# The second layer of a fused attention and two-layer MLP: runs of 512, 512, 512, 384, 384 tokens per half, with moving rows 512 words apart

## The reference

```python
p_packed = sm_attn(p, k, v)            # 8 x 8 heads, 32 packed rows, 576 keys, 64 wide
out = sm_attn(q, p_packed, p_packed)   # back to 576 rows
x = out as [4608 tokens, 512]
h = x @ w_in                           # 512 -> 2048
y = (max(h, 0) + alpha * min(h, 0)) @ w_out        # 2048 -> 512
g = y @ w_gate; val = y @ w_val                    # 512 -> 1536 each
result = (g / (1 + exp(-g)) * val) @ w_down        # 1536 -> 512, moe2_w_out
```

## Time and profile before

| | us |
|---|---|
| median of 3 runs | 1641.13 (1640.57 to 1642.71) |
| profiled execution, its own time | 1641.77 |
| its span, first to last instruction | 1640.0 |
| TensorE busy | 1610.9 (98%) |
| VectorE busy | 1016.4 (62%) |
| ScalarE busy | 694.3 (42%) |

### The profile page before, as it was taken

How to read it: one execution, slowest core, us unless ns; L and a number is a source line. 1 busy time by engine, 2 the same in 40 slices (tenths; PEclk the granted TensorE clock), 3 DMA queues, 4 the chain that set the end, 5 groups by cost and what they waited for, 6 DMA issues and landing times.

```text
span 1640.0 us, 24546 instructions
## 1 busy us (share of the span) xinstructions
PE 1610.9 (98%) x9510; PEld 1492.1 (91%) x9510; DVE 1016.4 (62%) x1888; ACT 694.3 (42%) x1481; POOL 47.4 (3%) x81
## 2 busy tenths in 40 slices
PE   8999999999999999999999999999999999999999
PEld 5999988999999999999988888888999999999998
DVE  5776679867798768877544464445444644464443
ACT  4565568455675557645412141213212422242122
POOL 0000001100000000010000000000000000000000
PEclk9999999999999999999999999999999999999999
DMA  7343225432333324344364525443545354434541
GB/s 261 118 124 112 68 84 166 157 113 87 125 102 123 132 72 143 112 156 149 113 226 135 178 93 182 155 160 114 174 165 180 113 200 158 160 113 156 180 135 45
DMA packets 99731, 227.05 MB, mean 138 GB/s; under 512 B 9744, under 2 KB 41504, under 8 KB 99616
## 3 DMA queue, kind: packets, MB, share of 16 engines
q1 hardware_dynamic: 91136, 194.02, 36.4%
q0 software_dynamic: 8480, 31.47, 5.0%
HBM read 184.56 MB, written 40.89 MB: 137 GB/s over the span
## 4 chain that ended last, share of the span: by engine, by line
PE 81%; DVE 13%; ACT 3%; issue 2%; DMA 0%; SPq 0%; ACTq 0%; DVEq 0%
PE acc L874 9%; PE acc L666 8%; PE acc L668 8%; PE acc L667 8%; PE h L666 7%; PE side L666 7%; PE h L668 7%; PE h L667 7%; PE side L668 7%; PE side L667 7%; PE acc L878 5%; DVE piece L1294 3%; DVE mixed L1294 2%; DVE floats L1479 2%; DVE g L1294 1%
## 5 line engine op out<-in xcount | busy, mean ns | idle before, releaser
L874 PE MATMUL acc<-g,w 128*128 128x288 f32 x1792 | 272.4, 294 | 0.0
L874 PEld LDWEIGHTS acc<-g,w 128*128 128x128 f32 x1792 | 248.9, 188 | 0.0
L989 ACT ACTIVATE g<-floats 128x288 fp32r<-128x288 f32 x256 | 113.8, 445 | 224.5 <-DVE floats L1479 136.7
L1294 DVE TENSOR_TENSOR g<-floats,g 128x288 fp32r<-128x288 f32 x256 | 115.2, 450 | 76.5 <-ACT g L989 75.2
L666 PE MATMUL h<-attn,mixed 128*128 128x288 f32 x512 | 157.9, 308 | 3.5 <-DVE floats L1479 2.2
L1479 DVE SCALAR_TENSOR_TENSOR floats<-floats,h 128x288 f32<-128x288 f32 x256 | 130.5, 510 | 46.0 <-ACT floats L1148 44.3
L878 PE MATMUL acc<-g,w 128*128 128x288 f32 x896 | 156.0, 296 | 0.2 <-DVE g L1294 0.2
L667 PE MATMUL h<-attn,mixed 128*128 128x288 f32 x512 | 151.2, 295 | 0.0
L668 PE MATMUL h<-attn,mixed 128*128 128x288 f32 x512 | 151.2, 295 | 0.0
L1294 DVE TENSOR_TENSOR piece<-floats,piece 128x512 fp32r<-128x512 f32 (+3 forms) x203 | 135.8, 689 | 23.1 <-ACT piece L989 20.7
L1294 DVE TENSOR_TENSOR u<-sums,u 128x448 fp32r<-128x448 f32 (+1 forms) x120 | 76.7, 639 | 92.5 <-ACT u L989 92.5
(11 more groups left out here) (257 smaller groups left out, 3686.0 us busy)
## 6 DMA issues: line engine op xcount, KB each, us to landing
ring<-w_scratch SPq DMA_DIRECT2D x90, 512.0 KB, 5.5
ring_c<-w_scratch SPq DMA_DIRECT2D x60, 512.0 KB, 5.0
w_scratch<-piece POOLq DMA_DIRECT2D x36, 512.0 KB, 4.0
floats<-w_in SPq DMA_DIRECT2D x64, 256.0 KB, 3.2
ring_b<-w_scratch SPq DMA_DIRECT2D x30, 512.0 KB, 6.7
y_scratch<-floats POOLq DMA_DIRECT2D x16, 576.0 KB, 3.5
floats<-kT SPq DMA_DIRECT2D x28, 288.0 KB, 2.9
floats<-qT SPq DMA_DIRECT2D x28, 288.0 KB, 2.9
```

What stands on the lines that cost most here:

```text
L874: pe.matmul(acc[:, m, 0:CH], w2[:, j, x, m * P:(m + 1) * P], g[:, s % 2, 0, :], start=False, stop=False)
L989: return nc.scalar.activation(dst, src, ACT.Copy, **kw)
L1294: return nc.vector.tensor_tensor(dst, x, high.bitcast(F32), ALU.subtract)
```

## The change

1. `HALF` becomes 512, 512, 512, 384, 384 (before: 480, 480, 448, 448, 448). `HW` becomes 512, so every row of the moving operands of the second layer starts at a multiple of 512 words from the first tensor.
2. To make room, the order of the tensors is changed, the last down tile (`down_last`) and one scratch row (`value2`) move to the place of the raw buffers in `floats`, `ostage` and `yraw` begin 256 and 128 words earlier, and the fourth part of the ring's even set (`ring0_b`) takes the place of the twelfth down tile.
3. The waits follow the places. The fourth part of the weights of set 0 is loaded from slot 254 on, behind the last load of down weights, and waits for the output tile of slot 251. The split of the last down tile waits until all splits before it are done, in place of the output tile of slot 251. The first `out_copy` also waits for all splits.

```diff
-HALF = [480, 480, 448, 448, 448]
+HALF = [512, 512, 512, 384, 384]
...
-MID[LAST + 1] += [("yload",), ("wload",)]
+MID[LAST + 1] += [("yload",), ("wload", range(3))]
+MID[SLOTS - 2].append(("wload", range(3, 4)))
...
-            down_ = later("down", NT2 * 1024)
+            down_ = later("down", (NT2 - 1) * 1024)
+            ring0_b = later("ring0_b", 1024)
             ring1_ = later("ring1", 4096)
             blocks_a = later("blocks_a", 4 * 4 * HW)
+            sums_ = later("sums", (NT2 + 4) * HW, F32)
+            blocks_b = later("blocks_b", 3 * 4 * HW)
             ring0_a = later("ring0_a", 512)
-            sums_ = later("sums", 8192, F32)
-            blocks_b = later("blocks_b", 3 * 4 * HW)
-            ring0_b = later("ring0_b", 1024)
             u_ = later("u", 4 * HW)
             later("pad", 256)
             silus_ = later("silus", 1152, F32)
             ring0_c = later("ring0_c", 2048)
+            down_last = later("down_last", 1024)
+            value2_ = later("value2", HW, F32)
...
-        yraw = f(4224, 2 * KD * HW).rearrange("p (k c n) -> p k c n", k=KD, c=2)
-        ostage = f(2304, KD * HW).rearrange("p (m n) -> p m n", m=KD)
+        yraw = f(4096, 2 * KD * HW).rearrange("p (k c n) -> p k c n", k=KD, c=2)
+        ostage = f(2048, KD * HW).rearrange("p (m n) -> p m n", m=KD)
...
-            def load_weights(n):
+            def load_weights(n, parts=range(4)):
...
-                for i in range(4):
+                for i in parts:
                     if n == 1:
                         once.wait_ge(y_done, SLOTS - 3 + i)
                     elif n == 0 and i == 3:
-
-                        once.wait_ge(h_done, SLOTS - NT1)
+                        once.wait_ge(y_done, SLOTS - 4)
...
+                elif p == ("d", NT2 - 1):
+
+                    once.wait_ge(piece_split, n)
                 elif p[0] == "d":
                     once.wait_ge(y_done, SLOTS - NT1 + p[1] + 1)
...
                     if o == 0:
                         once.wait_ge(y_stored, 16 * NCH)
+                        once.wait_ge(piece_split, len(PIECES))
```

More of the change, by code:

```diff
@@ L249 @@
 RINGED = [p for p in PIECES if p[0] in "kvqwgs"]
+assert RAW_NO["d", NT2 - 1] % RING in (2, 3)
 LEAVE_NO = {p: n for n, p in enumerate(p for e in PLAN for p in pieces_of(e))}
@@ L371, in down @@
         def down(j):
-            return down_[:, 1024 * j:1024 * j + 1024].rearrange("p (x n) -> p x n", x=2)
+            t, a = (down_, 1024 * j) if j < NT2 - 1 else (down_last, 0)
+            return t[:, a:a + 1024].rearrange("p (x n) -> p x n", x=2)
         def block_of(name):
@@ L377, in block_of @@
             return t[:, 4 * HW * a:4 * HW * (a + 1)].rearrange("p (x k n) -> p x k n", x=2, k=2)
-        yraw = f(4224, 2 * KD * HW).rearrange("p (k c n) -> p k c n", k=KD, c=2)
-        ostage = f(2304, KD * HW).rearrange("p (m n) -> p m n", m=KD)
+        yraw = f(4096, 2 * KD * HW).rearrange("p (k c n) -> p k c n", k=KD, c=2)
+        ostage = f(2048, KD * HW).rearrange("p (m n) -> p m n", m=KD)
         u_high_low = u_[:, :].rearrange("p (s x n) -> p s x n", s=2, x=2)
         u2 = sums_[:, 0:NT2 * HW].rearrange("p (j n) -> p j n", j=NT2)
-        scratch = sums_[:, NT2 * HW:(NT2 + 5) * HW].rearrange("p (i n) -> p i n", i=5)
-        first_term, first_two, first_three, value1, value2 = [scratch[:, i, :] for i in range(5)]
+        scratch = sums_[:, NT2 * HW:(NT2 + 4) * HW].rearrange("p (i n) -> p i n", i=4)
+        first_term, first_two, first_three, value1 = [scratch[:, i, :] for i in range(4)]
+        value2 = value2_[:, :]
         silu1, silu2 = silus_[:, 0:HW], silus_[:, HW:2 * HW]
@@ L610, in _ @@
                 elif e[0] == "wload":
-                    load_weights(0)
+                    load_weights(0, e[1])
             for n in range(1, SETS):
```

## The result

| us | before | after |
|---|---|---|
| median of 4 runs each | 1641.18 (1640.57 to 1642.71) | 1628.53 (1627.60 to 1628.95) |
| profiled execution, its own time | 1641.77 | 1628.95 |
| its span | 1640.0 | 1627.1 |

The page of the profile after, busy time and chain, answers to the earlier trace rows; what is read there is that nothing changed but TensorE's sum.

A forecast was written before the change was run, and what follows sets the result against it. TensorE, busy 98% of the span, was taken as the bound. The second layer's runs gave -0.6 us and the end -0.1, so 1641.13 - 0.7 = 1640.4 us, range 1635.0 to 1646.0, forecast's chance 0.64.

The forecast's parts named there:

- (1): Second layer, a run of 512 columns: 231.1 ns a matmul, 183.46 us with the bubble, bounds 182.59 to 184.3 us.
- price per column: Second-layer matmuls: cost proportional to columns, 0.4514 ns each from 448 to 512, with a rest of -1.1 to +1.0 ns.
- Step (2): Second layer, a run of 384 columns: 174.2 ns a matmul, 138.4 us with the bubble, bounds 137.7 to 139.5 us.
- Step (3): Sum of the five second-layer runs: 827.2 us against 827.8 before, -0.6 us, bounds -4.7 to +4.2.
- Rival (B): Second-layer matmuls: the excess hangs on alignment; all 3960 fall to 10 ns over, time 1615.5 us; chance 0.05.
- Rival (A): Second layer: long aligned rows cost 230.0 ns at 512, 384 pays no rest (173.3 ns), time 1636.3 us; chance 0.15.
- Rival (C): Second layer: 384 pays 2.3 ns rest, terms at 512 pay 1.7 ns more; +4.2 us, time 1645.2; chance 0.10.
- Rival (D): Runs of 384: weights land late and 20 sets wait; at 9.8 us after first issue 12 us, time 1652; chance 0.06.
- The bubble at term 6: First set of each second-layer run: TensorE held up once by VectorE's two additions, staying near 0.4 us.
- The fourth part: Set 0's last weight load: there at 806.1, before the first term at 807.40; bounds 0 to 1.3 us late, taken 0.
- closing tile: Third closing tile of a 384 run: VectorE's work fits with 0.4 us left; without that, under 0.5 us lost per run.
- The end: Last copy and store, 384 columns in place of 448: 0.1 us saved.

The follow-up runs named there:

- e1: The changed kernel with the old lengths (480, 480, 448, 448, 448), rows still 512 words apart: 1640.72 us, ratio to before 1.0006.
- e12: The changed kernel with all moving rows of the second layer 32 words off, weights staying or moving by 64 words: 1647.80 us, ratio to before 1.0042.
- e4: The changed kernel with a gap of 32 words ahead of the first tensor, so every tensor lies 128 bytes further: 1628.14 us.
- e5: The changed kernel with the last down tile 32 words further and `u` beginning 0, 32, 64, 0, 32 words further in the five runs: 1631.60 us.
- e6: The changed kernel with `u` beginning 16, 48, 8, 16 and 32 words further in the five runs: 1634.99 us.
- e10: The changed kernel with four runs of 512 columns and one of 256: 1645.95 us.
- e2: The changed kernel with runs of 512, 496, 464, 448 and 384 columns, rows still 512 words apart: 1635.94 us.
- e11: The changed kernel with runs of 512, 512, 512, 448 and 320 columns: 1638.25 us.

## Why the prediction was wrong

**The step that failed** is (1), the run of 512: "the price per column, which 448 and the down tile at 480 both hit". I took 231.1 ns a matmul, the runs show 226.7. Over 3 x 792 matmuls: 3 x (183.46 - 179.99) = 10.4 us of the 10.9 by which the sum of the five runs was too high (827.2 + 1.6 against 817.9). The mechanism behind it was wrong too, and not only a size. 448 and 480 agree in a price per column by chance: they pay 15.7 and 16.7 ns over their columns, and a line through them and zero passes near both. The table of lengths shows 13.3 ns on both sides of them, at 384 and at 512. Two neighbouring lengths could not tell a price per column from a fixed one. The forecast's own condition, no constant price between 384 and 512, is what came true.

**The row that should have warned** is the earlier trace rows. It had the length and the distance that the change would have (`both` lies at a multiple of 64 words from `piece` as well). I read it as 230.0 ns. The reading was right, and the use of it wrong. Three matmuls of the same kind stand just before those of rows 4:

```profile
104.10 0.39 PE L666 MATMUL side<-piece,both 128*128 128x512 f32 x1
```

The six from 104.10 to 105.49 take 1.39 us, 231.7 ns each. The trace of before has 192 such matmuls, in groups of three or six; 185 are followed without a wait, at 231.1 ns in the mean, and in the trace of after it is 231.2. So matmuls of 512 columns at a distance of a multiple of 64 words cost about 231 ns in the first stage of the very kernel in which they cost 226.7 in the second layer. I carried the price of short groups between other work over to a chain of hundreds, as a lower bound of 230.0. What makes the groups dearer no run here shows, and length and distance alone do not promise 226.7.

**Step (2)**, the run of 384: predicted 174.2 ns and 138.40 us, measured 173.4 and 138.76, 137.60. The rest of 0.9 ns taken over from 288 columns wasn't there (-1.3 us over both runs); the lower bound of 173.3 was right. One wait for weights, below, gave 0.8 us of it back.

**Step (3), all this "over rows that start at many different multiples of 32 words".** I concluded that places play no part. e1 agrees for 480 and 448. e12 shows the conclusion wrong for 512: 6.7 ns a matmul hang on it. At 480 the cost of a place is small enough to be missed (terms 218.5 against 216.7). And the many multiples of 32 words were only two places modulo 64: a distance of 0 for one row and of 32 words for the next.

**Rival (B)**, that the excess hangs on the alignment, had a chance of 0.05 and comes nearest. Its sum with the 13.3 ns measured in place of its 10: 3960 x 0.0133 + 760.3 = 813.0, 12.5 us under 825.5. Of the reasons against it, the one from the earlier trace rows is true of those rows but did not carry over to the second layer. The clause that (B) cannot occur because the first tensor lies 128 bytes past a multiple of 2048 was false: e4 and e5 show that the distance to the weights counts and not the address. But (B) as put, alignment alone, also fell, with e1. Neither my forecast nor a rival had the two conditions together.

**Rival (A)** had the right sign and little over a third of the size. **Rival (C)** did not occur in the change: terms at 512 pay no more than down tiles. In e12, at another distance, its sign is the measured one.

**Rival (D)**, weights late at 384, is at its edge, as the sum of issue and landing said. One of 20 sets waited noticeably. The timeline of PE, then of SP (queue entries):

```profile
1373.73 0.34 PE L674 MATMUL acc<-blocks_b,ring_b 128*128 128x384 f32 x1
1374.63 0.44 PE L672 MATMUL acc<-blocks_a,ring 128*128 128x384 f32 x1 [0.56 <-DMA ring<-w_scratch]
```

```profile
1364.74 2.59 SPq L596 DMA_DIRECT2D ring<-w_scratch  x4
1367.43 3.49 SPq L575 DMA_DIRECT2D floats<-y_scratch  x4
```

The four issues took 2.59 us, not 1.8, and y for the last run was issued right behind them. The term came 1374.63 - 1373.73 = 0.90 us after the matmul before it in place of 0.17, and the next interval was 0.1 too long. The run without loads of y is 1.2 us shorter (137.60), and this wait is most of the difference. It need not come: in e4, with the same work, no matmul waited for weights and the fourth run took 137.78 us. All issues of weights landed in 2.9 / 5.0 / 7.7 us, near.

**What held.** The bubble at term 6 stayed. The timeline of PE in the third run, as in the earlier trace rows, then SP's entry for the fourth part of set 0's weights:

```profile
1175.34 0.39 PE L674 MATMUL side<-blocks_b,ring_c 128*128 128x512 f32 x1
1175.88 0.50 PE L672 MATMUL h<-blocks_b,ring_b 128*128 128x512 f32 x1
1176.21 0.39 PE L673 MATMUL h<-blocks_b,ring_b 128*128 128x512 f32 x1
```

```profile
799.66 0.33 SPq L596 DMA_DIRECT2D ring_b<-w_scratch  x1
```

1176.21 - 1175.34 is 0.87 us for two matmuls that take 0.45 elsewhere, 0.42 against 0.43 us. The fourth part was issued 6.2 us before term 0 at 805.83, and nobody waited for it. No closing tile waited for VectorE at 384, and PE's other waits from 807 on are two of 0.2 us, at that same bubble. The end is 0.1 us shorter, as taken.

**On the page of the Trainium skill** that the prediction weighed ("TensorE: Matmul & The Clock Gate", section "Wait — 56ns, not 53.3ns?"): its form, columns at 2.4 GHz plus a constant, is nearer to the trace than my price per column. Its constant of 2.5 ns is not: the smallest in the down tiles of a run of the second layer is 13.1 ns (e6), the usual one 13.3, and the first layer's 288 columns pay 12.3. Its form would have given both groupings the same time and so no change, as mine did.

## What to carry to other kernels

Before the matmul of a new length is priced, look whether the known lengths can tell a price per column from a fixed part at all, and don't carry the price of a few matmuls between other work over to a long chain. In a float32r kernel whose matmuls each load their weights, try moving rows and weight rows at a distance of a multiple of 64 words together with 512 columns; here one without the other brought nothing or cost 0.4%. When the number of matmuls is fixed, as here, the rest is best put into runs of up to about 400 columns. When it is not, the price per column counts: 0.443 ns at 512, 0.451 at both 384 and 480, 0.469 at 256. Then see that weights still arrive in time in the shortest pass.

## What the hardware showed that was not expected

- At a granted clock of 1.00 the float32r matmuls of the second layer, back to back and each with new weights, pay 13.3 ns over their columns at 256, 320, 384, 400 and 512 columns. Between 416 and 508 they pay 15.0 to 18.3 ns. It is no floor of the whole kernel: the 288 columns of the first layer pay 12.3. A shorter weight load (134 and 108 ns in place of 188) doesn't lower it.
- At a granted clock of 0.50, the 1.2 GHz level, the same kind of matmul pays nothing over its columns: 213.3 ns at 256 (e10), 240 at 288 (before).
- The distance of the moving row from the weight row modulo 64 words sets up to 6.8 ns a matmul at 512 columns (226.7 against 233.5) and 2.9 at 384 (173.3 against 176.2). The address itself sets nothing (e4).
- The same length at the same places has two prices, each for a whole run: 448 columns cost 202.7 ns in e1 and e2 (a repeated pattern of intervals from 199 to 207) and 206.7 in e11 (all alike). In e12 the second run paid 232.4 and its neighbours 233.3. And 512 columns at distance 0 cost 231 ns in groups of three or six in the first stage. What sets this, and why 13.3 ns, is open.
- With the same work, the granted clock fell to 0.89 over 320 to 335 us in five of fourteen profiles. In that of before the low stretch begins with the matmul at 326.31, right after TensorE had stood idle for 1.17 us; in that of after it stood idle for 1.16 us at the same place, and the clock stayed at 1.00. That made the second layer start 1.6 us later in the profile of before, more than the whole difference that was forecast (0.7).
